# Matmul row 128 of a Fourier-MoE kernel moved to VectorE as an outer product

## The chip, the cores and the metric

The kernel runs on one core of a Trainium2 chip. The metric is the device time of one execution in microseconds. It is one program with five engines' instruction streams, ordered by semaphores that the author wrote by hand: TensorE (PE), VectorE (DVE), ScalarE (ACT), GpSimd (POOL) and SyncE (SP, which issues the DMAs).

## The reference

```
X = fft(fft(x, axis=1), axis=2).real          # x: 2 x 3008 x 256
h = X @ w_in1;  g = relu(h)**2;  y = g @ w_out1         # 256 -> 2048 -> 256
h = y @ w_in2
g = (a0 + a1*h + a2*h^2 + a3*h^3) / (1 + |b0|*|h| + |b1|*h^2 + 1e-6)
out = g @ w_out2                               # 6016 tokens
```

## The kernel before

The Fourier transform over 3008 is split into 47 and 64 points (stage 1, then `stage3` with twiddles); the transform over the 256 features is folded into `w_in1`. Tokens k and -k share their even part U and odd part V: with h1_plus = U-part and h1_minus = V-part, the two tokens' values are their sum and difference. So only 3012 columns of pairs are computed, in 12 tiles of 256 columns (`TILES`, `WIDE`; the last has 196), and each tile gives 512 tokens (the last 392).

The 128 rows of y that meet h1_plus are features 0 to 127. Feature 128 also belongs to the even part, but has no place in those 128 rows; it lies in row 0 of the odd half. Before the change it is a matmul of its own: `w_mid` and `y_mid` are 128-row tiles, zero but for three rows (weight low x y high, weight high x y high, weight high x y low). The zero rows are set by DVE (L637, L638), the three rows come by small DMAs (`load_mid`, L373, and L395), and row 0 of the odd half of `w_in1` is then zeroed by DVE (L653).

All products are done as high x high, low x high and high x low of values split in two (hi, lo), so each logical matmul is three.

The main loop has 96 steps s, 8 per tile (`UNITS`), each over two blocks of 128 of the 2048 hidden features. What the engines do in step s of the steady part, in this order:

- PE: `up1(s)` writes h1_minus (6 matmuls, L819) and h1_plus (8 matmuls, L830, two of them with w_mid) into PSUM banks 1 and 0; `down1(s-2)`; `up2(s-10)`; `down2(s-12)` (12 matmuls of 512 columns each).
- DVE: `add_and_subtract(s)` (L664, L665, reads bank 0 and the ACT copy of bank 1), `divide(s-11)` (L682, L684, L688), once in 8 steps `keep_z_lo` (L693), and `read_h2(s-10)` (L671, L672, L674).
- ACT: relu and square of unit s (L507, L509), once in 8 steps the z copy (L564), `from_h2(s-10)` (L525, L533), `keep_hi1(s)` (L516), once in 8 steps the output copy (L571), `abs_q` (L539), `keep_minus(s+1)` (L501), `seed_from_q` (L549, L552).
- POOL: `split2(s-11)` (L459, L461) and `keep_lo1(s)` (L452); before the loop it splits w_out1, w_in2 and w_out2 into hi and lo (L427, L429).
- SP: y of tiles 1 to 11 goes to DRAM in stage 3 and is read back tile by tile (L369) into one buffer, after the last `up1` of the tile before; outputs are stored.

Steps 0 to 9 lack up2 and down2 (the fill), and in them DVE also does the low part of the first g (`split1`, L703). After step 95 a tail of units without up1 is left. The last tiles of stage 3 (10 and 11) run within steps 0 and 1. `up1(m)` waits for the subtraction of m-1 (`diff_done`), `up2(m)` for `h2_read` of m-1, `add_and_subtract` for `plus_ready` and `minus_kept`.

Of the kernel before, what the change touches and what calls it, by code (L numbers as in the profile page):

```python
# [85 lines left out]
def tables():  # L86
# [43 lines left out]
def fft_moe_kernel(nc, x, w_in1, w_out1, w_in2, w_out2, coef, f47, fold, twiddle, out_t):  # L130
    y_hi_d = nc.dram_tensor("y_hi_dram", (DB, P, COLUMNS), F32, kind="Internal").ap()
    y_lo_d = nc.dram_tensor("y_lo_dram", (DB, P, COLUMNS), F32, kind="Internal").ap()

# [4 lines left out]
    with ctx:  # L138
# [42 lines left out]
        w_mid = sb("w_mid", [P, DFF], F32R)  # L181
        y_mid = sb("y_mid", [P, WIDE], F32R)
# [166 lines left out]
        def _(sp):  # L349
# [14 lines left out]
            load_w(w_out1_raw, w_out1, w_out1_loaded)  # L364

            def load_y(t):
                n = pairs(t)
                for v, s in zip(y_d, y_s):
                    sp.dma_start(s[:, :, 0:n].bitcast(F32), v[:, :, t * WIDE:t * WIDE + n]).then_inc(y_loaded, 16)  # L369

            def load_mid(t, hi, lo):
                for row, v in enumerate((hi, hi, lo)):
                    sp.dma_start(y_mid[row:row + 1, 0:pairs(t)].bitcast(F32), v).then_inc(y_mid_loaded, 16)  # L373
# [20 lines left out]
            for row, n in enumerate((1, 0, 0)):
                sp.dma_start(w_mid[row:row + 1, :].bitcast(F32), w_in1_s[n][0:1, 1, :].bitcast(F32)).then_inc(w_mid_loaded, 16)  # L395
            sp.wait_ge(y_lo_kept, 1)
            load_mid(0, *(s[0:1, 1, :].bitcast(F32) for s in y_s))
# [229 lines left out]
        def _(dve):  # L627
# [9 lines left out]
            dve.memset(w_mid[:, :].bitcast(F32), 0.0).then_inc(mid_zeroed, 1)  # L637
            dve.memset(y_mid[:, :].bitcast(F32), 0.0).then_inc(mid_zeroed, 1)  # L638
            for r in range(folds):
                sums, hi, lo = fold_views(r)  # L640
                dve.wait_ge(w_in1_hi, r + 1)
                nc.vector.tensor_tensor(lo, sums, hi.bitcast(F32), ALU.subtract).then_inc(w_in1_lo, 1)
            def keep_y_lo(t):
                hi, lo = y_tile(t)
                dve.wait_ge(y_hi_kept, t + 1)
                nc.vector.tensor_tensor(lo, uv_bank(t), hi.bitcast(F32), ALU.subtract).then_inc(y_lo_kept, 1)

            for t in range(EARLY):
# [1 line left out]
                if t == MID_AT:  # L650
                    dve.wait_ge(w_mid_loaded, 48)
                    for w in w_in1_s:
                        dve.memset(w[0:1, 1, :].bitcast(F32), 0.0).then_inc(mid_row_zeroed, 1)  # L653
# [283 lines left out]
```

## Time and profile before

| | us |
|---|---|
| median of 3 runs | 1047.09 (1045.85 to 1047.9) |
| the profiled execution | 1046.25 |
| its span, first to last instruction | 1044.5 |
| PE busy / weight loads | 1020.2 / 868.2 |
| ACT busy | 888.3 |
| DVE busy | 877.7 |
| POOL busy | 568.5 |
| mean granted TensorE clock | 0.990 |

Busy time of an engine is the union of its instructions' records. Matmuls overlap each other in the records, so how far apart two start says more than how long one is. The same holds for DVE and ACT to a smaller extent: an instruction can start a little before the record of the one ahead ends.

### The profile page before, as it was taken

How to read it: one execution, taken by the hardware profiler on the slowest of the kernel's cores; microseconds unless marked ns; L12 is line 12 of the kernel's file. 1: busy time of each engine (PE TensorE's matmuls, PEld its weight loads, DVE VectorE, ACT ScalarE, POOL GpSimd, SP SyncE). 2: the span in 40 equal slices, each digit the busy share in tenths (PEclk: the TensorE clock that was granted, in tenths of full speed). 3: DMA queues.
4: the chain of work that ended last, by engine and by line, in shares of the span. 5: the costliest groups of instructions: out<-in, count | busy, mean ns of one | idle time of the engine just before them, and what ended most of it. 6: DMA issues, size and time to landing. Idle time of an engine off the chain costs nothing.

```text
span 1044.5 us, 13875 instructions
## 1 busy us (share of the span) xinstructions
PE 1020.2 (98%) x5288; PEld 868.2 (83%) x5288; DVE 877.7 (84%) x839; ACT 888.3 (85%) x929; POOL 568.5 (54%) x303
## 2 busy tenths in 40 slices
PE   9999999999999999999999999999999999999985
PEld 8798878888888888888888888888888888888775
DVE  2455798988988988888888898898888898899997
ACT  2258888999999999999999999998998999898873
POOL 0226765565665655656556566465565565555352
PEclk9999999999999999999999999999999999999997
DMA  9765000001001001001001001001001001000000
GB/s 254 281 212 188 1 1 21 1 1 41 1 1 42 1 1 41 1 1 41 2 1 41 1 1 41 1 1 41 1 1 41 1 1 36 1 21 1 1 21 16
DMA packets 22580, 36.50 MB, mean 35 GB/s; under 512 B 1601, under 2 KB 17394, under 8 KB 21874
## 3 DMA queue, kind: packets, MB, share of 16 engines
q1 hardware_dynamic: 22514, 35.63, 10.4%
q8 instruction: 41, 0.67, 0.3%
q14 instruction: 25, 0.20, 0.1%
HBM read 23.78 MB, written 11.81 MB: 34 GB/s over the span
## 4 chain that ended last, share of the span: by engine, by line
PE 88%; DVE 6%; issue 3%; ACT 2%; DMA 0%; SPq 0%; DVEq 0%; ACTq 0%
PE ps L804 45%; PE ps L795 22%; PE ps L830 8%; PE ps L819 6%; PE ps L747 3%; PE ps L767 2%; PE ps L756 1%; DVE den_s L671 1%; DVE w_out_unsplit_lo L671 1%; DVE w_out_unsplit_lo L682 1%; DVE w_out_unsplit_lo L684 1%; DVE w_in_unsplit_hi L672 1%; ACT g_value L533 1%; PE ps L774 1%; DVE den_s L682 0%
## 5 line engine op out<-in xcount | busy, mean ns | idle before, releaser
L804 PE MATMUL ps<-g_hi,w_out_lo 128*128 128x512 f32 (+1 forms) x764 | 300.3, 393 | 15.5 <-POOL w_in_lo L461 8.8
L804 PE MATMUL ps<-g_hi,w_out_hi 128*128 128x512 f32 (+1 forms) x764 | 300.2, 393 | 0.0
L804 PE MATMUL ps<-g_lo,w_out_hi 128*128 128x512 f32 (+1 forms) x728 | 283.2, 389 | 0.0
L459 POOL CAST g_hi<-g_value 128x1024 fp32r<-128x1024 f32 x86 | 89.5, 1041 | 349.4 <-DVE g_value L688 349.4
L461 POOL TENSOR_TENSOR g_lo<-g_value,g_hi 128x1024 fp32r<-128x1024 f32 x86 | 207.6, 2414 | 6.9
L452 POOL TENSOR_TENSOR g_lo<-g_value,g_hi 128x1024 fp32r<-128x1024 f32 (+1 forms) x86 | 203.6, 2368 | 0.6 <-ACT g_hi L516 0.6
L804 PEld LDWEIGHTS ps<-g_hi,w_out_lo 128*128 128x128 f32 x764 | 145.5, 190 | 45.1 <-POOL w_in_lo L461 10.3
L804 PEld LDWEIGHTS ps<-g_hi,w_out_hi 128*128 128x128 f32 x764 | 145.1, 190 | 29.2
L671 DVE SCALAR_TENSOR_TENSOR den_s<-den_s,b_abs,ps 128x1024 f32<-128x1024 f32 x88 | 112.7, 1281 | 61.7 <-ACT g_value L533 61.5
L804 PEld LDWEIGHTS ps<-g_lo,w_out_hi 128*128 128x128 f32 x728 | 137.4, 189 | 25.5
L682 DVE SCALAR_TENSOR_TENSOR den_s<-den_s,seed_s 128x1024 f32<-128x1024 f32 x87 | 110.9, 1275 | 28.7 <-ACT seed_s L552 28.7
L539 ACT ACTIVATE den_s<-den_s 128x1024 f32<-128x1024 f32 x88 | 93.5, 1063 | 38.0 <-DVE den_s L671 38.0
L525 ACT ACTIVATE den_s<-ps,coef_s 128x1024 f32<-128x1024 f32 x88 | 98.2, 1116 | 25.9 <-PE ps L795 24.6
L795 PE MATMUL ps<-z_hi,w_in_lo 128*128 128x512 f32 x352 | 110.5, 395 | 2.9 <-DVE g_value L674 2.7
L688 DVE SCALAR_TENSOR_TENSOR g_value<-g_value,coef_s,den_s 128x1024 f32<-128x1024 f32 x86 | 110.5, 1285 | 3.0
L674 DVE SCALAR_TENSOR_TENSOR g_value<-g_value,coef_s,ps 128x1024 f32<-128x1024 f32 x86 | 110.1, 1280 | 3.0
L795 PE MATMUL ps<-z_lo,w_in_hi 128*128 128x512 f32 x352 | 109.4, 392 | 0.0
L795 PE MATMUL ps<-z_hi,w_in_hi 128*128 128x512 f32 x352 | 109.2, 392 | 0.0
L684 DVE SCALAR_TENSOR_TENSOR den_s<-den_s,seed_s 128x1024 f32<-128x1024 f32 x87 | 106.6, 1225 | 3.0
L507 ACT ACTIVATE g_value<-g_value 128x1024 f32<-128x1024 f32 (+1 forms) x96 | 100.1, 1043 | 8.2 <-DVE g_value L665 8.2
L672 DVE TENSOR_TENSOR g_value<-g_value,ps 128x1024 f32<-128x1024 f32 x86 | 104.4, 1213 | 0.0
L533 ACT ACTIVATE g_value<-ps,coef_s 128x1024 f32<-128x1024 f32 x86 | 103.3, 1201 | 0.0
(105 smaller groups left out, 1895.8 us busy)
## 6 DMA issues: line engine op xcount, KB each, us to landing
x_s<-x SPq DMA_DIRECT2D x16, 384.0 KB, 7.3
out_t<-out_s SPq DMA_DIRECT2D x11, 512.0 KB, 3.0
w_out_unsplit_lo<-w_out SPq DMA_DIRECT2D x2, 2048.0 KB, 17.7
tw_s<-twiddle SPq DMA_DIRECT2D x1, 3012.0 KB, 18.2
y_hi_dram<-y_stage_hi SPq DMA_DIRECT2D x10, 256.0 KB, 3.0
y_lo_dram<-y_stage_lo SPq DMA_DIRECT2D x10, 256.0 KB, 3.2
y_hi<-y_hi_dram SPq DMA_DIRECT2D x10, 256.0 KB, 2.8
y_lo<-y_lo_dram SPq DMA_DIRECT2D x10, 256.0 KB, 3.0
```

The source lines that it names most:

```text
L452: nc.gpsimd.tensor_tensor(g1_lo_s[:, p, :, 0:n], r_s[:, p, :, 0:n], g1_hi_s[:, m % 2, :, 0:n].bitcast(F32), ALU.subtract).then_inc(pool_lo ...
L461: nc.gpsimd.tensor_tensor(lo, g, hi.bitcast(F32), ALU.subtract).then_inc(g2_lo, 1)
L507: nc.scalar.activation(r, r, ACT.Relu).then_inc(relu_done, 1)
L533: nc.scalar.activation(num_of(m), h2_banks(m)[:, :, 0:width(m)], ACT.Identity, bias=a2, scale=a3).then_inc(cubic_done, 1)
L671: nc.vector.scalar_tensor_tensor(den, den, b_abs[:, 0:1], h2, ALU.add, ALU.mult).then_inc(q_signed, 1)
L672: nc.vector.tensor_tensor(num, num, h2, ALU.mult).then_inc(t_h_done, 1)
L674: nc.vector.scalar_tensor_tensor(num, num, a1, h2, ALU.add, ALU.mult).then_inc(h2_read, 1)
L682: nc.vector.scalar_tensor_tensor(den, den, Q_CONST, seed, ALU.add, ALU.mult).then_inc(t_done, 1)
L684: nc.vector.scalar_tensor_tensor(den, den, 2.0, seed, ALU.subtract, ALU.mult, reverse0=True).then_inc(rec_done, 1)
L688: nc.vector.scalar_tensor_tensor(num, num, a0, den, ALU.add, ALU.mult).then_inc(g2_done, 1)
L795: last = nc.tensor.matmul(h[:, i, 0:n], lhs, rhs, start=(j == 0), stop=(j == len(products) - 1))
L804: last = nc.tensor.matmul(acc[:, mb, 0:n], w[a][:, f, mb * P:(mb + 1) * P], g[c][:, i, 0:n], start=(f == 0 and j == 0), stop=(f == FB - 1 ...
```

## The change

Feature 128 leaves the matmuls. Its row of y (called u) and of w_in1 (2048 values, turned to a column of 128 per block, `w_col`) are kept in exact form; DVE writes their outer product for unit m into bank 0, and the six matmuls of h1_plus that are left add onto it (start=False).

- PE: `up1` has 6 + 6 matmuls in place of 6 + 8. Ahead of h1_minus it waits for `minus_kept` (ACT's copy), ahead of h1_plus for `outer_ready`. In stage 3, behind tile 7, one small matmul sums hi and lo of the w row into the column.
- DVE: two `tensor_scalar` of 128x256 per unit, with a per-partition scalar from `w_col`, SBUF to PSUM. They stand directly behind `add_and_subtract(s)` in steps 0 to 10, later behind `divide` and ahead of `keep_z_lo` and `read_h2`. In stage 3 a one-row copy of u per tile, ahead of the low part of y, and the copy of the column. The memsets L637, L638 and L653 go.
- POOL: two memsets of 1x2048 (the zero rows of w_in1), behind the split of w_out1 and ahead of the wait for w_in2.
- ACT: one DMA issue in stage 3.
- SP: in place of the `w_mid`/`y_mid` DMAs, two stores of the w row, one store of u per tile (1 KB), one broadcast load of u per tile to 128 partitions; y has two buffers, tile 1 is loaded at the end of stage 3 ahead of w_in2, and tile t+1 behind the last up1 of tile t-1.

```diff
+            def outer_product(m):
+                t, n = m // UNITS, pairs(m // UNITS)
+                if m % UNITS == 0:
+                    dve.wait_ge(u_loaded[t % Y_BUFS], 16 * (t // Y_BUFS + 1))
+                after(dve, diff_done, m)
+                for i in range(2):
+                    f = 2 * (m % UNITS) + i
+                    nc.vector.tensor_scalar(h1_plus(m)[:, i, :], u_s[:, t % Y_BUFS, 0:n], w_col[:, f:f + 1], None, ALU.mult
+                                            ).then_inc(outer_ready, 1)
...
                 add_and_subtract(s)
+                if before is None:
+                    outer_product(s + 1)
...
                     divide(before)
+                if before is not None and unit(s + 1) is not None:
+                    outer_product(s + 1)
                 if summed is not None and summed % UNITS == UNITS - 1:
                     keep_z_lo(summed // UNITS)
...
             def up1(m):
-                after(pe, diff_done, m)
+                after(pe, minus_kept, m)
...
-                if m % UNITS == 0:
-                    pe.wait_ge(y_mid_loaded, 48 * (t + 1))
+                pe.wait_ge(outer_ready, 2 * m + 2)
...
-                    products = [(w_in1_s[1][:, 0, f], y_s[0][:, 0, 0:n]), (w_in1_s[0][:, 0, f], y_s[1][:, 0, 0:n]),
-                                (w_mid[:, f], y_mid[:, 0:n]), (w_in1_s[0][:, 0, f], y_s[0][:, 0, 0:n])]
-                    for j, (lhs, rhs) in enumerate(products):
-                        last = nc.tensor.matmul(h1_plus(m)[:, i, :], lhs, rhs, start=(i == 0 and j == 0), stop=(j == 3),
+                    for a, c in ((1, 0), (0, 1), (0, 0)):
+                        last = nc.tensor.matmul(h1_plus(m)[:, i, :], w_in1_s[a][:, 0, f], y_s[c][:, 0, 0:n],
+                                                start=False, stop=(a, c) == (0, 0), skip_group_check=True)
...
+            pool.wait_ge(w_row_stored, 32)
+            for w in w_in1_s:
+                pool.memset(w[0:1, 1, :].bitcast(F32), 0.0).then_inc(mid_row_zeroed, 1)
...
             for t in range(1, TILES):
                 sp.wait_ge(plus_ready, t * UNITS)
-                after_stored(sp, t)
-                load_y(t)
-                load_mid(t, *(v[0:1, 1, t * WIDE:t * WIDE + pairs(t)] for v in y_d))
+                if t + 1 < TILES:
+                    load_u(t + 1)
+                    load_y(t + 1)
```

## Rows read from the trace of the kernel before

**Rows 1.** Page: engines' busy time; the chain that ended last, by engine.

```profile
PE 1020.2 (98%) x5288; PEld 868.2 (83%) x5288; DVE 877.7 (84%) x839; ACT 888.3 (85%) x929; POOL 568.5 (54%) x303
...
PE 88%; DVE 6%; issue 3%; ACT 2%; DMA 0%; SPq 0%; DVEq 0%; ACTq 0%
```

**Rows 2.** Windows: stretch, length, busy of PE, PEld, DVE, ACT, POOL; clock; DMA.

```profile
140.00:160.00 20.00, 18.09 (x80) 14.62 (x79) 17.67 (x16) 17.21 (x18) 11.70 (x7) 0.91 0.00 0
...
500.00:600.00 100.00, 99.95 (x504) 84.43 (x503) 88.90 (x83) 91.96 (x93) 57.83 (x31) 1.00 0.03 11
```

**Rows 3.** PE by form, then timeline (start, duration) of two successive steps.

```profile
L830 PE MATMUL ps<-y_mid,w_mid 128*128 128x256 f32 x176 | 49.1, 279 | 0.0
...
609.92 0.28 PE L830 MATMUL ps<-y_mid,w_mid 128*128 128x256 f32 x1
610.04 0.28 PE L830 MATMUL ps<-y_hi,w_in_hi 128*128 128x256 f32 x1
...
619.85 0.28 PE L830 MATMUL ps<-y_mid,w_mid 128*128 128x256 f32 x1
```

**Rows 4.** DVE timeline, steady steps, one with z; idle before in brackets.

```profile
499.08 1.28 DVE L671 SCALAR_TENSOR_TENSOR den_s<-den_s,b_abs,ps 128x1024 f32<-128x1024 f32 x1 [0.92 <-ACT g_value L533]
...
504.28 1.23 DVE L682 SCALAR_TENSOR_TENSOR den_s<-den_s,seed_s 128x1024 f32<-128x1024 f32 x1 [0.26 <-ACT seed_s L552]
...
506.80 1.28 DVE L688 SCALAR_TENSOR_TENSOR g_value<-g_value,coef_s,den_s 128x1024 f32<-128x1024 f32 x1
508.00 1.22 DVE L693 TENSOR_TENSOR z_lo<-ps,z_hi 128x1024 fp32r<-128x1024 f32 x1
509.98 1.28 DVE L671 SCALAR_TENSOR_TENSOR den_s<-den_s,b_abs,ps 128x1024 f32<-128x1024 f32 x1 [0.76 <-ACT g_value L533]
...
519.37 1.28 DVE L671 SCALAR_TENSOR_TENSOR den_s<-den_s,b_abs,ps 128x1024 f32<-128x1024 f32 x1 [0.40 <-ACT g_value L533]
```

**Rows 5.** DVE timeline in the tail: a short instruction with per-partition scalar.

```profile
1033.76 0.63 DVE L688 SCALAR_TENSOR_TENSOR w_in_unsplit_hi<-w_in_unsplit_hi,coef_s,w_out_unsplit_lo 128x392 f32<-128x392 f32 x1
1034.30 0.97 DVE L698 TENSOR_TENSOR w_in_hi<-w_in_unsplit_hi,g_hi 128x784 fp32r<-128x784 f32 x1
```

**Rows 6.** DVE timeline: a 256-wide memset; two 512-wide instructions without such a scalar.

```profile
38.06 0.27 DVE L638 MEMSET y_mid<- 128x256 f32 x1
...
502.73 0.68 DVE L664 TENSOR_TENSOR g_value<-ps,minus_s 128x512 f32<-128x512 f32 x1
503.33 0.68 DVE L665 TENSOR_TENSOR g_value<-ps,minus_s 128x512 f32<-128x512 f32 x1
```

**Rows 7.** DVE timeline: an L682 while GpSimd still works.

```profile
464.60 1.27 DVE L682 SCALAR_TENSOR_TENSOR den_s<-den_s,seed_s 128x1024 f32<-128x1024 f32 x1 [0.26 <-ACT seed_s L552]
465.91 1.23 DVE L684 SCALAR_TENSOR_TENSOR den_s<-den_s,seed_s 128x1024 f32<-128x1024 f32 x1
```

**Rows 8.** DVE timeline, steps of the narrow last tile.

```profile
944.76 1.28 DVE L671 SCALAR_TENSOR_TENSOR den_s<-den_s,b_abs,ps 128x1024 f32<-128x1024 f32 x1 [0.17 <-ACT g_value L533]
...
949.86 1.25 DVE L682 SCALAR_TENSOR_TENSOR den_s<-den_s,seed_s 128x1024 f32<-128x1024 f32 x1 [0.42 <-ACT seed_s L552]
...
952.40 1.28 DVE L688 SCALAR_TENSOR_TENSOR g_value<-g_value,coef_s,den_s 128x1024 f32<-128x1024 f32 x1
953.93 1.28 DVE L671 SCALAR_TENSOR_TENSOR den_s<-den_s,b_abs,ps 128x1024 f32<-128x1024 f32 x1 [0.24 <-ACT g_value L533]
```

**Rows 9.** Timelines of the fill: ACT's copy in two steps; PE's wait for tile 1.

```profile
85.77 0.58 ACT L501 ACTIVATE minus_s<-ps 128x512 f32<-128x512 f32 x1
...
89.88 0.58 ACT L501 ACTIVATE minus_s<-ps 128x512 f32<-128x512 f32 x1
...
102.50 0.39 PE L819 MATMUL ps<-y_hi,w_in_lo 128*128 128x256 f32 x1 [0.69 <-DMA y_lo<-y_lo_dram]
```

**Rows 10.** GpSimd timeline: end of the w_out1 split, start and end of the later splits.

```profile
57.77 2.35 POOL L429 TENSOR_TENSOR w_out_lo<-w_out_unsplit_lo,w_out_hi 128x1024 fp32r<-128x1024 f32 x1
87.27 1.04 POOL L427 CAST w_in_hi<-w_in_unsplit_lo 128x1024 fp32r<-128x1024 f32 x1 [27.15 <-DMA w_in_unsplit_lo<-w_in]
...
119.12 2.40 POOL L429 TENSOR_TENSOR w_out_lo<-w_out_unsplit_lo,w_out_hi 128x1024 fp32r<-128x1024 f32 x1
```

More of the change, by code:

```diff
@@ L48 @@
 MID_AT = 3
+Y_BUFS = 2
 WIDE = 2 * BATCH * N2
@@ L127, in column_of_token, with fft_moe_kernel @@
     return column
-def fft_moe_kernel(nc, x, w_in1, w_out1, w_in2, w_out2, coef, f47, fold, twiddle, out_t):
+def fft_moe_kernel(nc, x, w_in1, w_out1, w_in2, w_out2, coef, f47, fold, twiddle, pair, out_t):
     y_hi_d = nc.dram_tensor("y_hi_dram", (DB, P, COLUMNS), F32, kind="Internal").ap()
     y_lo_d = nc.dram_tensor("y_lo_dram", (DB, P, COLUMNS), F32, kind="Internal").ap()
+    u_d = nc.dram_tensor("u_dram", (1, COLUMNS), F32, kind="Internal").ap()
+    w_row_d = nc.dram_tensor("w_row_dram", (2, DFF), F32, kind="Internal").ap()
     out_v = out_t.rearrange("(k p) n -> p k n", p=P)
@@ L179, in kept_and_rest @@
             return value, sb(f"{name}_lo", [P, bufs, 2, TN], F32R)
-        w_mid = sb("w_mid", [P, DFF], F32R)
-        y_mid = sb("y_mid", [P, WIDE], F32R)
+        u_s = sb("u_s", [P, Y_BUFS, WIDE])
+        w_rows = sb("w_rows", [2 * FB, P])
+        pair_s = sb("pair_s", [2 * FB, FB])
+        w_col = sb("w_col", [P, FB])
+        with ExitStack() as transform:
+            u_stage = sb("u_stage", [1, STAGE_BUFS + 1, WIDE], stack=transform)
+        y_odd = [sb(f"y_odd_{n}", [P, DB, WIDE], F32R) for n in ("hi", "lo")]
+        sb("to_w_in2", [P, DFF + WIDE - Y_BUFS * WIDE - 2 * DB * WIDE - P - 2 * FB])
         w_in2_s, (_, w_in2_raw) = weights("w_in2", [P, DB, DFF])
@@ L364, in _, with store_u, load_u @@
             load_w(w_out1_raw, w_out1, w_out1_loaded)
+            after(sp, s1_ready, S1_GROUPS)
+            sp.dma_start(pair_s[:, :], pair).then_inc(pair_loaded, 16)
             def load_y(t):
                 n = pairs(t)
[L368 to L373, printed above, removed]
+                for v, s in zip(y_d, y_of(t)):
+                    sp.dma_start(s[:, :, 0:n].bitcast(F32), v[:, :, t * WIDE:t * WIDE + n]
+                                 ).then_inc(y_loaded[t % Y_BUFS], 16)
+            def store_u(t):
+                n = t % (STAGE_BUFS + 1)
+                sp.wait_ge(u_kept, t + 1)
+                sp.dma_start(u_d[:, t * WIDE:t * WIDE + pairs(t)], u_stage[:, n, 0:pairs(t)]).then_inc(u_stored[n], 16)
+            def load_u(t):
+                n = pairs(t)
+                after_u_stored(sp, t)
+                sp.dma_start(u_s[:, t % Y_BUFS, 0:n], u_d[:, t * WIDE:t * WIDE + n].to_broadcast([P, n])
+                             ).then_inc(u_loaded[t % Y_BUFS], 16)
             def store_out(t):
@@ L390, in store_y @@
                                  ).then_inc(y_stored[(t - 1) % STAGE_BUFS], 16)
-            sp.wait_ge(mid_zeroed, 2)
             sp.wait_ge(w_in1_lo, folds)
[L394 to L397, printed above, removed]
+            for n in range(2):
+                sp.dma_start(w_row_d[n:n + 1, :], w_in1_s[n][0:1, 1, :].bitcast(F32)).then_inc(w_row_stored, 16)
+            store_u(0)
             for t in range(1, TILES):
+                store_u(t)
                 store_y(t)
+                if t <= Y_BUFS:
+                    load_u(t - 1)
             for t in range(TILES - STAGE_BUFS, TILES):
                 after_stored(sp, t)
+            for t in range(TILES - STAGE_BUFS - 1, TILES):
+                after_u_stored(sp, t)
+            load_y(1)
             load_w(w_in2_raw, w_in2, w_in2_loaded)
@@ L649, in _ @@
                 keep_y_lo(t)
[L650 to L653, printed above, removed]
+                if t == COLUMN_AT + 1:
+                    dve.wait_ge(w_col_summed, 1)
+                    nc.vector.tensor_copy(w_col[:, :], ps[:, FOLD_BANKS[2], 0:FB]).then_inc(w_col_ready, 1)
+                    dve.wait_ge(w_col_ready, 1)
+                    outer_product(0)
             dve.wait_ge(coef_loaded, 16)
@@ L786, in _ @@
                 stage3(t)
+                if t == COLUMN_AT:
+                    pe.wait_ge(w_in1_lo, folds)
+                    pe.wait_ge(pair_loaded, 16)
+                    pe.wait_ge(w_rows_loaded, 16)
+                    nc.tensor.matmul(ps[:, FOLD_BANKS[2], 0:FB], w_rows[:, :], pair_s[:, :], start=True, stop=True
+                                     ).then_inc(w_col_summed, 1)
             def up(h, w, src, m, n, ready):
```

33 lines of the change are left out of this document (23 added, 10 removed).

## Prediction

> **What bounds the kernel now.** I read the page first: PE is busy in 98% of the span and makes up 88% of the chain that ended last, against 84% and 85% for DVE and ACT [rows 1]. Then the windows: from about 160 to 900 us PE is busy all the time (99.95 of 100 us at clock 1.00), DVE 88.9, ACT 92.0 [rows 2]. Then the timelines, for the spacing. The same matmul of two successive steps starts 9.93 us apart (9.92 over many steps), and two neighbours of 256 columns 0.12 us apart [rows 3]. DVE shows how near the next limit is. From L671 to L682 it takes 5.20 us (through ACT's abs, copy, ln and exp), from L682 to L688 2.52, and behind L688 the next instruction starts 1.20 later if nothing holds it: 8.92 us. Then it waits for ACT before L671, 0.92 us in the usual step [rows 4]. ACT's own loop, where it is not held by PE, brings L671 every 9.39 us (509.98 to 519.37) [rows 4]. So there are three rings side by side: PE 9.92, ACT 9.39, and DVE with ACT's seed in it 8.92. The tail behind step 95 is DVE's, back to back, and the change adds nothing there.
>
> **What goes on PE.** Two of 14 short matmuls per unit, 192 in all (176 of them 256 wide) [rows 3]. 2 x 0.12 = 0.24 us per step: PE's ring becomes 9.68. The wait that moved from the subtraction to ACT's copy comes earlier than the old one, so it costs nothing.
>
> **What comes on DVE, and where.** Two `tensor_scalar` of 256 columns with a per-partition scalar stand between L688 and L671, so they lie in the 8.92 ring, not beside it. The 0.92 us of waiting before L671 covers them only until the ring is longer than PE's. No row shows such an instruction, nor any DVE write to PSUM. What one takes of DVE's time is the distance to the next start. For instructions with such a scalar it is 1.20 us at 1024 columns [rows 4] and 0.54 at 392 [rows 5], so 1.044 ns per column, and 0.54 - 136 x 0.001044 = 0.40 us at 256. Without the scalar 512 columns take 0.60 [rows 6]; by the same slope 256 take 0.33. The low end is the memset of 256 columns, which reads nothing: 0.27 [rows 6]. The high end is a PSUM write that takes away the overlap with the next instruction: the 0.63 record at 392 [rows 5] less 0.14 gives 0.49. So the pair costs 0.54 to 0.98, and I take 0.80, from the nearest rows in kind (same scalar operand, same engine).
>
> One rule of the Trainium skill bears on it. Its page "Vector Engine (DVE) Microarchitecture Reference", section "Measured stream behaviour on trn2", gives 1.0417 ns per column and about 75 ns per instruction, whatever the op; that is an estimate of 0.34 each, 0.68 the pair. The slope agrees with this trace, but the rows with a per-partition scalar show some 0.06 us more.
>
> **Steady steps.** DVE's ring is 8.92 + 0.80 = 9.72, against PE's 9.68: DVE takes over as the bound. Once in 8 steps z_lo stands in the same ring; its record is 1.22 [rows 4], its slot 0.08 less, 1.14. The mean is 9.72 + 1.14/8 = 9.86, against 9.92: 0.06 us gained per step. The z copy of ACT (about 0.9) and its output copy (0.3 late at L539 now) run beside the longer DVE part and cost nothing more. PE's phase changes too: up2 of the next unit waits for L674, which ends 3.73 after L671, and the way from there round PE is 9.68, so it is no ring of its own. Another edge is GpSimd: where L682 comes early behind the L688 before, it overlaps the last GpSimd subtraction and takes 1.27, and L684 starts 1.31 later in place of 1.26 [rows 7]. That was 7.08 us behind L688; with 0.80 it is 1.20 + 0.80 + 5.20 = 7.20, so about nothing; with 0.67 it is 7.07 and costs 0.05 per step. 96 steps less 14 of fill and 8 narrow ones are 74: -4.4 us.
>
> **Narrow tile.** Steps now take 9.17 (944.76 to 953.93). DVE's ring: 5.10 + 2.54 [rows 8] + 1.20, and two instructions of 196 columns, 0.34 each: 9.52. Six steps lose 0.34, 2.0 us; the first and the one with z_lo gain about 0.3 together. +1.7 us.
>
> **Fill.** Steps 1 to 10 are PE's: ten times 0.24 gained, if ACT's loop lets it. That brings the minus copy every 4.11 us [rows 9], against PE's 4.46 now and 4.22 after, so it just does. DVE has over a microsecond idle per step there; the pair hides. The second y buffer takes away PE's wait of 0.69 us for tile 1 [rows 9]; later tiles' loads were hidden anyway. -3.1 us. Then two steps (10 to 12) are already ruled by the ACT ring of 9.39 and will be by DVE's 9.72: +0.7. The w column's small matmul stands on PE in stage 3, about 0.3 (one matmul behind a wait took 0.39 [rows 9]). Hidden: the DVE memsets that go (PE had other work), the row copies of u (DVE idles 1.1 us per tile in stage 3), and SP's extra issues, some 1.7 us per tile of stage 3 against 1.79 that PE gives it. GpSimd ends the w_out1 split at 60.1 us [rows 10]; two memsets of 2048 columns, 1.8 each on DVE, end near 64, ahead of the first up1 at 66.7. The w_in2 load is issued some 1 us later and shares the DMA engines with tile 1, so the split that starts at 87.3 and ends at 121.5 [rows 10] ends 2 to 3 us later; PE needs it at 123 to 125 and has waits for `h2_read` behind it that take up what is left. Sum of the start: -2.1 us.
>
> The clock was granted at 0.91 over 140 to 160 us [rows 2], about 2 us lost in a stretch at the lower level behind a wait of PE; I leave it as it is, within 2 us either way.
>
> **Sum.** -4.4 + 1.7 - 2.1 = -4.8 us. Against the profiled execution's 1046.25 that is 1041.5; the median of the runs is 0.84 above it, so 1042.3. I say 1042. Each 0.01 us on the pair moves it by 0.8 us; from 0.86 on nothing is gained.
>
> **Rivals.**
> - The pair costs as instructions without a scalar, 0.67. Ring 9.59 and 0.05 for GpSimd, with z_lo 9.78: -0.14 x 74 = -10.4; narrow +1.3, start -2.3: 1035.7. For it: the same slope, and one tensor input less. Against: all three kinds of rows with a scalar are dearer.
> - PE stays the bound: the pair is 0.62 or less ((9.68 - 1.14/8) - 8.92), as it would be if one instruction did two columns per cycle (0.40 less 0.13 is 0.27 each, 0.53). -0.24 x 74, narrow -1.8, start -2.8: 1024.7. For it: the memset's 0.27. Against: no row of DVE is faster than one column per cycle but by a few per cent. The skill's page "VectorE: DVE Perf Modes", section "The perf-mode tier table", gives fp32 `tensor_scalar` twice the rate in SBUF, and not with an operand in PSUM; where that cap did not hold for the destination, this would be the result.
> - Slower: a write to PSUM does not overlap the next instruction. The pair is 0.98, the ring 9.90, with z_lo 10.04: +0.12 x 74 = +8.9; narrow 9.68 a step, +2.8; start -1.7: 1057. It decides from 0.88 per pair. For it: nothing in the trace shows a PSUM write by DVE. Against: reading PSUM or SBUF makes no difference to the distance (L671 and L688 both 1.20).
> - The zero rows on GpSimd are late, or the split of w_in2 is: if a memset of one row took four times DVE's 1.8 us, up1(0) would start at 74 and not at 66.7. With the rest as forecast: 1049.
>
> **How the numbers follow.** What a measurement of this kernel can tell from no change is about 0.2%, 2.1 us. Forecast 0.44, pair as without scalar 0.24, PE-bound 0.07, slower by the PSUM write 0.15, late start 0.03; the rest, 0.07, is a pair between 0.83 and 0.88. Faster: 0.24 + 0.07 + 0.39 = 0.70; same 0.12 (that rest and the upper edge of the forecast); slower 0.18. The range goes from 1030 to 1053: it holds the forecast, the cheaper pair, and the near half of the slower case, and leaves out PE-bound and the dearest pairs. The likeliest case's own range is 1039 to 1045.
>
> **What would show it.** In the steady steps: L671 without idle time ahead of it (0.92 to about 0), 9.7 us between two of them and 10.86 across a z_lo; the two new instructions at 0.40 us distance; PE idle 0.05 to 0.2 us per step, released by DVE's outer product or by L674, and busy no longer 99.9%. Up1 with 12 matmuls in 1.43 us. In the fill no wait for y_lo at tile 1, and first up2 done some 3 us sooner. In the narrow tile 9.5 us per step. A pair at 0.34 us distance or less, or PE without idle time, would show the forecast wrong on the fast side; more than 0.43, on the slow side.

## The result, and the profile after

| | before | after |
|---|---|---|
| median, us | 1046.7 (1045.42 to 1047.9, 8 runs) | 1043.12 (1040.07 to 1044.19, 8 runs) |
| ratio | | 0.9961 [0.9947, 0.9975] |
| the profiled execution / its span | 1046.25 / 1044.5 | 1043.1 / 1041.3 |

The forecast was 1042. The time fits, but partly by luck: two of its terms are wrong by 6.1 and 4.7 us, with opposite signs. Most of what follows is about them.

In the kernel after, L671, L672, L674 are L725, L726, L728; L664 and L665 are L718 and L719; L682, L684, L688 are L736, L738, L742; `keep_z_lo` is L747 and the outer product L690. PE's up1 is L884 and L892, up2 L859, down L868. GpSimd's split of g is L498, L500, L491, its split of the weights L463, L465; ACT's L533 is L575.

The page (busy time by engine, then the chain by engine) answers to [rows 1]: PE 17 us less, DVE 64 more, and the chain is no longer PE's.

```profile
PE 1003.2 (96%) x5098; PEld 848.1 (81%) x5098; DVE 941.8 (90%) x1040; ACT 882.0 (85%) x929; POOL 572.1 (55%) x305
...
DVE 45%; ACT 28%; issue 15%; PE 9%; POOL 2%; DMA 1%; DVEq 0%; ACTq 0%; SPq 0%
```

Windows (columns as in [rows 2]). The first is a stretch in which PE now stands still; the others answer to [rows 2].

```profile
120.00:140.00 20.00, 12.98 (x52) 10.41 (x51) 18.11 (x16) 15.84 (x18) 16.19 (x9) 0.74 0.00 0
140.00:160.00 20.00, 20.00 (x101) 16.91 (x100) 17.60 (x21) 16.81 (x18) 11.58 (x6) 1.00 0.00 1
500.00:600.00 100.00, 98.66 (x486) 82.58 (x485) 96.23 (x103) 91.82 (x95) 59.04 (x31) 1.00 0.05 13
```

DVE's timeline in two steady steps, the second with a z_lo; it answers to [rows 4]. The two halves of the outer product are one row (x2).

```profile
486.75 1.28 DVE L742 SCALAR_TENSOR_TENSOR g_value<-g_value,coef_s,den_s 128x1024 f32<-128x1024 f32 x1
487.95 0.87 DVE L690 TENSOR_SCALAR ps<-u_s,w_col 128x256 f32<-128x256 f32 x2
488.73 1.27 DVE L725 SCALAR_TENSOR_TENSOR den_s<-den_s,b_abs,ps 128x1024 f32<-128x1024 f32 x1
...
493.91 1.23 DVE L736 SCALAR_TENSOR_TENSOR den_s<-den_s,seed_s 128x1024 f32<-128x1024 f32 x1 [0.27 <-ACT seed_s L594]
...
498.41 1.27 DVE L725 SCALAR_TENSOR_TENSOR den_s<-den_s,b_abs,ps 128x1024 f32<-128x1024 f32 x1
...
508.10 1.21 DVE L747 TENSOR_TENSOR z_lo<-ps,z_hi 128x1024 fp32r<-128x1024 f32 x1
509.23 1.27 DVE L725 SCALAR_TENSOR_TENSOR den_s<-den_s,b_abs,ps 128x1024 f32<-128x1024 f32 x1
```

From L690 to L725 it is 0.78 us: the pair's price. L725 has no idle time ahead of it (0.92 before), and steps are 9.68 to 9.70 apart, 10.82 across the z_lo. A tile of eight steps takes 78.7 us, where it took 79.6.

PE's own spacing must be read beside this. In the usual step the first matmul of up1 starts 9.70 us after that of the step before (mean of these steps, 170 to 885 us), so PE and DVE are equally long. Once per tile PE plainly waits for DVE: the z_lo makes L728 late, and up2 of the next tile waits for it. In most tiles this step is 10.74 on PE, and the two starts at the wait are 1.07 apart in place of 0.23 (PE's timeline of the kernel after):

```profile
590.75 0.40 PE L868 MATMUL ps<-g_hi,w_out_hi 128*128 128x512 f32 x1
591.82 0.47 PE L859 MATMUL ps<-z_hi,w_in_lo 128*128 128x512 f32 x1 [0.67 <-DVE g_value L728]
```

The whole difference can be laid out on one instruction. In the two traces the first instruction of `read_h2` of steps 13, 87 and 94 and of the last unit starts at (before: L671, after: L725):

```profile
150.75 1.28 DVE L671 SCALAR_TENSOR_TENSOR den_s<-den_s,b_abs,ps 128x1024 f32<-128x1024 f32 x1 [1.33 <-ACT g_value L533]
887.36 1.28 DVE L671 SCALAR_TENSOR_TENSOR den_s<-den_s,b_abs,ps 128x1024 f32<-128x1024 f32 x1 [0.92 <-ACT g_value L533]
...
1026.71 1.02 DVE L671 SCALAR_TENSOR_TENSOR w_out_unsplit_lo<-w_out_unsplit_lo,b_abs,ps 128x784 f32<-128x784 f32 x1
```

```profile
154.79 1.28 DVE L725 SCALAR_TENSOR_TENSOR den_s<-den_s,b_abs,ps 128x1024 f32<-128x1024 f32 x1
882.34 1.27 DVE L725 SCALAR_TENSOR_TENSOR den_s<-den_s,b_abs,ps 128x1024 f32<-128x1024 f32 x1
949.87 1.27 DVE L725 SCALAR_TENSOR_TENSOR den_s<-den_s,b_abs,ps 128x1024 f32<-128x1024 f32 x1
1022.62 1.03 DVE L725 SCALAR_TENSOR_TENSOR w_out_unsplit_lo<-w_out_unsplit_lo,b_abs,ps 128x784 f32<-128x784 f32 x1
```

(Step 94 before: 953.93, in [rows 8].)

| stretch | before | after | difference | forecast |
|---|---|---|---|---|
| start, to step 13 | 150.75 | 154.79 | +4.0 | -2.1 |
| 74 steady steps | 736.61 | 727.55 | -9.1 | -4.4 |
| narrow steps, 87 to 94 | 66.57 | 67.53 | +1.0 | +1.7 |
| behind that, to the end of the span | 90.6 | 91.4 | +0.9 | 0 |
| span | 1044.5 | 1041.3 | -3.2 | -4.8 |

**The start, up to step 10.** The first `read_h2` (step 10) starts at 121.21 before and at 121.22 after, where the forecast had it 2.8 us earlier (3.1 for the fill less 0.3 for the column's matmul). The first up1 starts 1.19 later: stage 3 began 0.67 later (49.59 in place of 48.92; in the other versions, whose code is the same up to there, it begins at 49.19 to 50.18), and the column's matmul takes about 0.4 of PE. The next three steps, with the last two tiles of stage 3 in them, take 13.66 in place of 12.58. DVE works from 74.4 to 82.6 us without a gap, with the pair and the copies of u added, and PE waits for it twice:

```profile
76.62 0.39 PE L892 MATMUL ps<-y_hi,w_in_lo 128*128 128x256 f32 x1 [0.64 <-DVE ps L690]
78.66 0.50 PE L868 MATMUL ps<-g_hi,w_out_lo 128*128 128x512 f32 x1 [1.06 <-DVE g_lo L757]
```

From there to up1 of step 10 the forecast holds: 30.07 in place of 32.22.

**The start, from step 10 on.** DVE, GpSimd and PE between 124 and 135 us of the kernel after (start, duration; idle before in brackets):

```profile
126.41 1.97 DVE L736 SCALAR_TENSOR_TENSOR den_s<-den_s,seed_s 128x1024 f32<-128x1024 f32 x1 [0.27 <-ACT seed_s L594]
128.41 3.25 DVE L738 SCALAR_TENSOR_TENSOR den_s<-den_s,seed_s 128x1024 f32<-128x1024 f32 x1
131.69 1.28 DVE L742 SCALAR_TENSOR_TENSOR g_value<-g_value,coef_s,den_s 128x1024 f32<-128x1024 f32 x1
132.90 0.87 DVE L690 TENSOR_SCALAR ps<-u_s,w_col 128x256 f32<-128x256 f32 x2
```

```profile
124.91 2.38 POOL L465 TENSOR_TENSOR w_out_lo<-w_out_unsplit_lo,w_out_hi 128x1024 fp32r<-128x1024 f32 x1
127.25 3.32 POOL L491 TENSOR_TENSOR g_lo<-g_value,g_hi 128x1024 fp32r<-128x1024 f32 x1
```

```profile
133.82 0.58 PE L892 MATMUL ps<-y_odd_hi,w_in_lo 128*128 128x256 f32 x1 [5.50 <-DVE ps L690]
```

Two things meet here. GpSimd's weight split, which ended at 121.5 before [rows 10], now ends at 127.3, in the middle of the first `divide`. L736 and L738 both read two tensors in SBUF, as do L465 and L491, and none of the two on DVE gets done while one of the two on GpSimd is at work: L736 lasts 0.74 us longer than its usual 1.23 and ends 1.1 behind L465, L491 lasts 3.32 in place of 2.4, and L738 3.25, ending 1.1 behind L491. And the outer product of unit 12 is the first that stands behind a `divide` in place of directly behind the subtraction, so PE, which needs it for up1 in step 12, stands still for 5.5 us with the down products queued behind (just ahead of this it had already waited 1.52 us for L465); the granted clock is 0.74 in that window, and behind the wait the matmuls of 256 columns start 0.21 apart in place of 0.12: the lower of the two levels, 1.2 GHz.

The Trainium skill, page "SBUF — State Buffer", section "Who interferes with whom", has this as a rule: a VectorE instruction with two SBUF inputs and a GpSimd instruction that reads SBUF exclude each other for the whole of an instruction, and whoever is issued first goes on. The four rows agree with it.

### The profile page after: what moved, and what is told of

It reads as the page before. It is cut to its first block, busy times and chain, and to the rows that moved or that the text cites. A ratio compares the mean times of both kernels' runs of the same rounds, so it can differ in the third digit from the quotient of the medians.

```text
span 1041.3 us, 13708 instructions
## 1 busy us (share of the span) xinstructions
PE 1003.2 (96%) x5098; PEld 848.1 (81%) x5098; DVE 941.8 (90%) x1040; ACT 882.0 (85%) x929; POOL 572.1 (55%) x305
## 4 chain that ended last, share of the span: by engine, by line
DVE 45%; ACT 28%; issue 15%; PE 9%; POOL 2%; DMA 1%; DVEq 0%; ACTq 0%; SPq 0%
DVE den_s L725 9%; DVE den_s L738 9%; DVE den_s L736 9%; ACT seed_s L594 9%; ACT seed_s L591 8%; DVE g_value L742 8%; ACT minus_s L543 5%; DVE ps L690 4%; PE ps L805 3%; PE ps L825 2%; PE ps L814 1%; ACT g_value L575 1%; PE ps L868 1%; ACT g_value L549 1%; POOL w_in_lo L465 1%
## 5 line engine op out<-in xcount | busy, mean ns | idle before, releaser
L868 PE MATMUL ps<-g_hi,w_out_lo 128*128 128x512 f32 (+1 forms) x764 | 301.6, 395 | 17.3 <-POOL w_in_lo L500 8.0
L868 PE MATMUL ps<-g_hi,w_out_hi 128*128 128x512 f32 (+1 forms) x764 | 300.3, 393 | 0.0
L868 PE MATMUL ps<-g_lo,w_out_hi 128*128 128x512 f32 (+1 forms) x728 | 283.9, 390 | 0.0
L498 POOL CAST g_hi<-g_value 128x1024 fp32r<-128x1024 f32 x86 | 89.6, 1042 | 339.5 <-DVE g_value L742 339.5
L500 POOL TENSOR_TENSOR g_lo<-g_value,g_hi 128x1024 fp32r<-128x1024 f32 x86 | 207.3, 2411 | 6.9
L491 POOL TENSOR_TENSOR g_lo<-g_value,g_hi 128x1024 fp32r<-128x1024 f32 (+1 forms) x86 | 204.6, 2380 | 0.0
L868 PEld LDWEIGHTS ps<-g_hi,w_out_lo 128*128 128x128 f32 x764 | 145.9, 191 | 47.3 <-POOL w_in_lo L500 9.3
L868 PEld LDWEIGHTS ps<-g_hi,w_out_hi 128*128 128x128 f32 x764 | 145.2, 190 | 29.2
L868 PEld LDWEIGHTS ps<-g_lo,w_out_hi 128*128 128x128 f32 x728 | 137.9, 189 | 25.6
L736 DVE SCALAR_TENSOR_TENSOR den_s<-den_s,seed_s 128x1024 f32<-128x1024 f32 x87 | 107.7, 1238 | 25.3 <-ACT seed_s L594 25.3
L859 PE MATMUL ps<-z_hi,w_in_lo 128*128 128x512 f32 x352 | 110.7, 395 | 8.4 <-DVE g_value L728 8.4
L725 DVE SCALAR_TENSOR_TENSOR den_s<-den_s,b_abs,ps 128x1024 f32<-128x1024 f32 x88 | 112.1, 1273 | 5.3 <-ACT g_value L575 5.0
L742 DVE SCALAR_TENSOR_TENSOR g_value<-g_value,coef_s,den_s 128x1024 f32<-128x1024 f32 x86 | 110.5, 1285 | 3.0
L728 DVE SCALAR_TENSOR_TENSOR g_value<-g_value,coef_s,ps 128x1024 f32<-128x1024 f32 x86 | 110.2, 1281 | 3.0
L738 DVE SCALAR_TENSOR_TENSOR den_s<-den_s,seed_s 128x1024 f32<-128x1024 f32 x87 | 108.6, 1249 | 3.0
L859 PE MATMUL ps<-z_lo,w_in_hi 128*128 128x512 f32 x352 | 109.0, 391 | 0.0
L859 PE MATMUL ps<-z_hi,w_in_hi 128*128 128x512 f32 x352 | 108.6, 390 | 0.0
L726 DVE TENSOR_TENSOR g_value<-g_value,ps 128x1024 f32<-128x1024 f32 x86 | 104.5, 1215 | 0.0
L575 ACT ACTIVATE g_value<-ps,coef_s 128x1024 f32<-128x1024 f32 x86 | 103.1, 1199 | 0.0
## 6 DMA issues: line engine op xcount, KB each, us to landing
w_in_raw<-w_in SPq DMA_DIRECT2D x1, 2048.0 KB, 10.5
```

The source lines that it names most:

```text
L491: nc.gpsimd.tensor_tensor(g1_lo_s[:, p, :, 0:n], r_s[:, p, :, 0:n], g1_hi_s[:, m % 2, :, 0:n].bitcast(F32), ALU.subtract).then_inc(pool_lo ...
L500: nc.gpsimd.tensor_tensor(lo, g, hi.bitcast(F32), ALU.subtract).then_inc(g2_lo, 1)
L575: nc.scalar.activation(num_of(m), h2_banks(m)[:, :, 0:width(m)], ACT.Identity, bias=a2, scale=a3).then_inc(cubic_done, 1)
L725: nc.vector.scalar_tensor_tensor(den, den, b_abs[:, 0:1], h2, ALU.add, ALU.mult).then_inc(q_signed, 1)
L726: nc.vector.tensor_tensor(num, num, h2, ALU.mult).then_inc(t_h_done, 1)
L728: nc.vector.scalar_tensor_tensor(num, num, a1, h2, ALU.add, ALU.mult).then_inc(h2_read, 1)
```

## Experiments

All changes are against the kernel after. Each ratio is against a before measured in the same series: 1047.31 for the load moved, the pair moved in every step, 14 matmuls and the pair twice; 1046.51 for the others. Where a time is set against the kernel after (1043.12), the two come from different series, whose befores lie within 0.8 us.

### The load of w_in2 ahead of tile 1

```diff
@@ SP, end of stage 3
+            load_w(w_in2_raw, w_in2, w_in2_loaded)
+            load_w(w_out2_raw, w_out2, w_out2_loaded)
             load_y(1)
-            load_w(w_in2_raw, w_in2, w_in2_loaded)
-            load_w(w_out2_raw, w_out2, w_out2_loaded)
```

> SP issues the loads of w_in2 and w_out2 ahead of the load of y tile 1; all else as changed. Theory A (the start is lost by the late split of w_in2 and w_out2 on GpSimd, which ends at 127.3 us where it ended at 121.5 before, holds DVE in the first divide for 2.8 us and then PE for 5.5): the w_in2 load is issued 1 us earlier and doesn't share its time with y; it landed 6.3 us later than before, of which 2.9 come from the last store of y and remain. The split ends at about 124.5; the first L742 comes about 2 us earlier; 1040 to 1042, 1 to 3 us faster than the changed kernel. Rival B (the load's lateness comes from stage 3 ending late alone): no difference. Rival C: y of tile 1 now comes late and PE waits for it: it is needed at 102 us and would land at about 98, so no.

Measured 1038.08 (1037.21 to 1039.16), ratio 0.9914 [0.99, 0.9927]: more than theory A's 1040 to 1042. The load of w_in2 is issued only 0.3 us earlier (83.33), but the split starts at 90.77 in place of 93.60 and ends at 125.3; step 13's L725 comes at 152.94, 1.85 earlier than in the kernel after. DVE's timeline: L736 still meets the end of L491 (at 127.67), L738 is free.

```profile
127.26 1.49 DVE L736 SCALAR_TENSOR_TENSOR den_s<-den_s,seed_s 128x1024 f32<-128x1024 f32 x1 [0.27 <-ACT seed_s L594]
128.78 1.23 DVE L738 SCALAR_TENSOR_TENSOR den_s<-den_s,seed_s 128x1024 f32<-128x1024 f32 x1
```

PE still waits, 4.78 us, for the outer product:

```profile
132.16 0.58 PE L892 MATMUL ps<-y_odd_hi,w_in_lo 128*128 128x256 f32 x1 [4.78 <-DVE ps L690]
```

So the late split is one part of the start's loss: PE's 1.52 us for L465 is gone and the wait of 5.50 is 0.72 shorter, but most of that wait stays. The span is 3.9 us shorter, and 1.9 of that is this. The other 2.0 lies behind the last L725, where nothing was changed and the clock was higher (0.86 from 1020 to 1040 us, 0.66 after the change). Whether that is chance stays open: all four runs here show a mean clock of 0.992 or 0.993, and only two of the eight of the kernel after show 0.992, at 1040.1 and 1040.3 us. So the 5.0 us between the medians is explained for 1.9.

### The outer product directly behind the subtraction in every step

```diff
                 add_and_subtract(s)
-                if before is None:
+                if unit(s + 1) is not None:
                     outer_product(s + 1)
...
-                if before is not None and unit(s + 1) is not None:
-                    outer_product(s + 1)
```

> The outer product stands directly behind add_and_subtract in every step, not behind divide. Theory A (the steady step is DVE's ring L725 to L725, 8.91 + 0.78 = 9.69): DVE waits there 0.27 us for ACT's seed, and behind the difference the pair begins 0.1 later because it waits for its end; the way from L725 to L736 becomes 4.23 + 0.72 + 0.78 = 5.73 in place of 5.19 and the pair is gone from the rest, 9.45 in all, with z_lo 9.59: less than PE's 9.68. PE is the bound, -0.16 us x 74 steps and some in the narrow tile: 1030 +- 3. Rival (PE is the bound already, and its 9.68 is met by the 9.69): no change, 1043. Rival (the position matters since PE gets its outer product too late): the same gain, but then PE's idle time before up1 in the changed kernel would be seen behind the outer product, and the trace shows it behind L728.

Measured 1033.57 (1033.07 to 1034.18), ratio 0.987 [0.9857, 0.9884], just above the range of 1030 +- 3. PE's long wait is gone, and DVE's usual steady steps are 9.64 apart: the pair now runs while ACT makes the seed for L736, where DVE had waited 0.27. DVE's timeline of a steady step, and GpSimd's of the same:

```profile
566.18 0.68 DVE L719 TENSOR_TENSOR g_value<-ps,minus_s 128x512 f32<-128x512 f32 x1
566.90 0.88 DVE L690 TENSOR_SCALAR ps<-u_s,w_col 128x256 f32<-128x256 f32 x2
567.68 1.40 DVE L736 SCALAR_TENSOR_TENSOR den_s<-den_s,seed_s 128x1024 f32<-128x1024 f32 x1
569.12 1.23 DVE L738 SCALAR_TENSOR_TENSOR den_s<-den_s,seed_s 128x1024 f32<-128x1024 f32 x1
```

```profile
565.58 2.43 POOL L491 TENSOR_TENSOR g_lo<-g_value,g_hi 128x1024 fp32r<-128x1024 f32 x1
```

The expected ring of 9.45 isn't reached: L736 would come before L491 ends at 568.0, and lasts 1.40 until 1.1 behind that. L742 releases GpSimd's split of g, and the split's last part holds L736: with DVE it forms a ring of its own, of 9.64. That is less than PE's spacing, 9.69 in seven of eight steps, so PE is the bound in those, as theory A had it. The 4.9 us that 74 steady steps gain (722.7 in place of 727.6) come for the most part from the step with the z_lo: on PE it takes 10.2 to 10.5 now, where it took 10.74 in most tiles.

### Both

The two edits together.

> Loads of w_in2 and w_out2 ahead of y tile 1, and the outer product directly behind the difference in every step. If the two gains are of different places (start, steady steps) they add: 1043 - 5 - 9.5 = 1028.5. If both mend the same loss at the start (DVE's first divide held by GpSimd's late split, and PE waiting for the outer product behind it), part is counted twice: 1031 to 1033. Steady steps as in the run with the product behind the difference, 9.64 with L736 at 1.40 us.

Measured 1031.23 (1030.91 to 1031.95), ratio 0.9854 [0.984, 0.9867]: the fastest complete version, and faster than before and after. The first `divide` is no longer held, and the window in which PE stood still reads:

```profile
120.00:140.00 20.00, 18.52 (x94) 15.29 (x93) 18.28 (x20) 18.85 (x20) 12.78 (x7) 1.00 0.00 1
```

From the first L725 to that of step 13 the traces show 29.5 us before, 33.6 after, 30.9 with the load moved, 30.9 with the pair moved, 28.7 with both. So each edit takes away 2.7 and both together 4.9: nearly additive in this stretch, and the two causes account for all of the 4.0 that it had lost. They do nothing for the 2.8 that failed to be gained ahead of it (first L725 at 121.43). Steady steps are as with the pair moved alone (722.7 us for 74). The time as a whole is not additive (1028.5 was expected for that). In the traces most of what is missing lies behind step 94, where the load moved is 2.0 shorter than the kernel after, the pair moved 0.5, and both 1.0.

### Only unit 12's outer product moved

```diff
-                if before is None:
+                if before is None or before == 0:
                     outer_product(s + 1)
...
-                if before is not None and unit(s + 1) is not None:
+                if before is not None and before > 0 and unit(s + 1) is not None:
```

> Only the outer product of unit 12 (step 11) goes directly behind the difference instead of behind the first divide; all else as changed. Theory (PE waits 5.5 us there since this product stands behind the first divide, which waits for the first seed and for GpSimd; the clock then falls): PE's wait goes, the clock stays at 1.00 in 120 to 140 us, 2 to 4 us gained, 1039 to 1041; the steady steps unchanged at 9.69. Rival (the start is bound by GpSimd's late split in any case): PE waits for GpSimd instead, under 1 us gained.

Measured 1040.78 (1039.81 to 1041.63), ratio 0.9945 [0.9933, 0.9957]. PE's 5.5 us wait splits into smaller ones (1.8 for the weight split, 1.3 for L491, 1.4 for the outer product of unit 13, which still stands behind its `divide`), the clock in 120 to 140 us is still 0.83, and the stretch from the first L725 to step 13 is 32.0 in place of 33.6. The rest of the wait had only been covered by it: L738 is held for 3.27 here too. Moving one instance takes 1.6 us; moving those behind it too takes 2.7 with the split just as late (the run with every pair moved). The time is the one expected, but the theory's own signs, no wait of PE and a clock of 1.00, are not there: the rival is right that PE then waits for GpSimd, though it had the gain at under 1 us.

### Two of the removed matmuls back on PE

```diff
-                    for a, c in ((1, 0), (0, 1), (0, 0)):
+                    for a, c in ((1, 0), (1, 0), (0, 1), (0, 0)):
```

One product per block is added twice, so h1_plus is wrong by that product; PE has 14 short matmuls per unit as before.

> As changed, but one of the six h1_plus products per block is issued twice, so PE has 14 short matmuls per unit again (the low-by-high product is added twice). Theory A: PE's ring is 9.92 again against DVE's 9.69 (9.83 with z_lo): PE the bound, 0.09 us x 74 = +6.5 us against the changed kernel, 1049 to 1051. Then the kernel's gain in the steady part needs both sides, and DVE takes the pair in for nothing. Rival (DVE's pair is the cost of the step and PE's work is beside it): no difference, 1043.

Measured 1052.93 (1052.65 to 1053.25), ratio 1.0055 [1.0041, 1.0069], 9.8 us above the kernel after and above the 1049 to 1051 of theory A. Windows and DVE's timeline:

```profile
500.00:600.00 100.00, 99.98 (x502) 84.44 (x501) 95.55 (x103) 91.39 (x94) 58.36 (x30) 1.00 0.04 13
```

```profile
503.02 0.87 DVE L690 TENSOR_SCALAR ps<-u_s,w_col 128x256 f32<-128x256 f32 x2
504.03 1.28 DVE L725 SCALAR_TENSOR_TENSOR den_s<-den_s,b_abs,ps 128x1024 f32<-128x1024 f32 x1
```

PE is the bound again: steps of 9.93, a tile of 79.7 (79.6 before), and 0.23 us of slack between the pair and L725. So the pair is nearly hidden in the steady part as long as PE has 14 matmuls (737.8 us for 74 steps, 736.6 before), and the 9 us that the steady part gained come from the two matmuls. It cost more than the 6 to 8 expected for the same reason that the forecast's steady term was too small (below).

### The pair twice

Each `tensor_scalar` is issued a second time with the same operands, behind a wait for its first issue; only the second signals PE.

> As changed, but each of the two tensor_scalar is issued twice (same result). Theory A: ring 9.69 + 0.78 + a little for the wait = 10.5 to 10.55; +0.8 x 82 steps: +66 us, 1106 to 1112. Rival (PE is still the bound, DVE has slack of some tenths): +0.78 less the slack; with 0.1 of slack +58 us or less.

Measured 1108.09 in one run. L690 and the repeated L695 start at 507.05 and 507.83, the next L730 (this kernel's `read_h2`) at 508.60; steps are 10.46 apart, 9.69 plus 0.77. What is added on DVE in this place adds the same to the step, with nothing to hide it. Together with the 14 matmuls this says that neither engine has slack in the kernel after: more work on either makes the step longer.

### No pair

```diff
-                for i in range(2):
+                for i in range(0):
...
-                pe.wait_ge(outer_ready, 2 * m + 2)
+                after(pe, diff_done, m)
...
-                                                start=False, stop=(a, c) == (0, 0), skip_group_check=True)
+                                                start=(i == 0 and (a, c) == (1, 0)), stop=(a, c) == (0, 0), skip_group_check=True)
```

Feature 128's product is left out altogether, and PE's first product starts the sum.

> As changed without the two tensor_scalar (feature 128's product is left out of the result); PE waits for the subtraction ahead of h1_plus instead. Theory A: DVE's ring is 8.91, PE the bound at 9.68 with no idle time: 0.16 us x 74 below the changed kernel, narrow tile 0.3 x 6 too, and PE has no wait of 5.5 us in step 12: 1043 - 12 - 2 - 3 = 1026. It is the floor for any place of the pair. Rival (something else holds the steady step at 9.69): 1040.

Measured 1031.78 (1031.48 to 1031.9), ratio 0.9858 [0.9844, 0.9871]. The floor of 1026 is not there. From the first L725 to step 13 it takes 32.3 us, 2.7 more than before: without any pair, the late split still holds L738 for 3.27, and PE waits 1.67 and 1.61 for GpSimd. The steady part gains 5.7 where 12 was expected, because PE's step with the z_lo stays at 10.2 (9.69 in the others). DVE's timeline has slack again, and two steps are still 9.70 apart:

```profile
483.92 1.28 DVE L725 SCALAR_TENSOR_TENSOR den_s<-den_s,b_abs,ps 128x1024 f32<-128x1024 f32 x1 [0.52 <-ACT g_value L575]
...
493.62 1.28 DVE L725 SCALAR_TENSOR_TENSOR den_s<-den_s,b_abs,ps 128x1024 f32<-128x1024 f32 x1 [0.57 <-ACT g_value L575]
```

That is PE's ring with 12 short matmuls, forecast at 9.68. The 74 steady steps take 721.9 us, against 722.7 with the pair directly behind the subtraction: there the pair is all but free, and moving it gets back 4.9 of the 5.7 us that the pair costs the steady part in its place behind the `divide`. This run also shows what the pair costs in the fill: up1 of step 3 starts 12.56 us behind the first one, and 13.66 in the kernel after.

### The pair as one instruction

```diff
-                for i in range(2):
-                    f = 2 * (m % UNITS) + i
-                    nc.vector.tensor_scalar(h1_plus(m)[:, i, :], u_s[:, t % Y_BUFS, 0:n], w_col[:, f:f + 1], None, ALU.mult
-                                            ).then_inc(outer_ready, 1)
+                f = 2 * (m % UNITS)
+                nc.vector.tensor_tensor(h1_plus(m), u_s[:, t % Y_BUFS, 0:n].unsqueeze(1).to_broadcast([P, 2, n]),
+                                        w_col[:, f:f + 2].unsqueeze(2).to_broadcast([P, 2, n]), ALU.mult
+                                        ).then_inc(outer_ready, 2)
```

> The two tensor_scalar become one tensor_tensor of 2x256 (u repeated over the blocks, the column value repeated along the row), at the same place behind divide. Theory A1 (only the sum on DVE counts): 0.60 us as other 512-wide rows in place of 0.78, ring 9.51, 1.5 us per tile: -14, PE-bound at about 1031. Theory A2 (an instruction with two SBUF inputs shuts GpSimd's reads out and is shut out by them, as L736 was at 1.40 us in the run with the product behind the difference): GpSimd's cast starts 1.35 behind L742 and now waits for the tensor_tensor until 1.80, its chain of 5.85 us ends at 7.65 and not at 7.20, and L736, ready at 6.99, lasts 1.8 us: ring 9.65 to 9.7, no gain. A broadcast operand that is read slower would show as a record above 0.68.

Measured 1062.02 (1061.28 to 1064.41), ratio 1.0145 [1.0129, 1.016]: slower than either theory. The instruction itself is the cheaper one. DVE's and GpSimd's timelines:

```profile
489.07 0.69 DVE L689 TENSOR_TENSOR ps<-u_s,w_col 128x512 f32<-128x512 f32 x1
489.68 1.27 DVE L725 SCALAR_TENSOR_TENSOR den_s<-den_s,b_abs,ps 128x1024 f32<-128x1024 f32 x1
...
494.87 1.73 DVE L736 SCALAR_TENSOR_TENSOR den_s<-den_s,seed_s 128x1024 f32<-128x1024 f32 x1 [0.27 <-ACT seed_s L594]
```

```profile
489.22 1.44 POOL L498 CAST g_hi<-g_value 128x1024 fp32r<-128x1024 f32 x1 [3.73 <-DVE g_value L742]
490.74 2.41 POOL L500 TENSOR_TENSOR g_lo<-g_value,g_hi 128x1024 fp32r<-128x1024 f32 x1
493.12 2.40 POOL L491 TENSOR_TENSOR g_lo<-g_value,g_hi 128x1024 fp32r<-128x1024 f32 x1
```

It takes 0.61 us in place of 0.78. But it has two inputs in SBUF and starts 0.15 us ahead of GpSimd's cast, which waits it out (1.44 in place of 1.04); L491 ends at 495.5 and not at 494.0 as in the kernel after (0.9 of the 1.5 because the whole step lies that much later), and L736, which needs two SBUF inputs too, lasts 1.73 until 1.1 behind it. The step is 10.03: 0.17 saved, 0.51 lost. Theory A2 named this mechanism and nearly the record (1.8), but its terms don't add up to its sum: 6.99 until L736 is ready, 1.8 for it and 1.26 for L738 make 10.05, and not 9.65 to 9.7.

## Why the prediction came out, point by point

- **The pair, 0.80.** Right: 0.78, 0.39 each. The rival without scalar cost (0.67) and the one with no overlap after a PSUM write (0.98) are both refuted; a 256-column `tensor_scalar` to PSUM overlaps the next instruction as others do.
- **DVE takes over, ring 9.72.** Right for DVE's ring: 9.69, with L725 following L690 at once, and 10.82 across z_lo (forecast 10.86). But PE's, forecast at 9.68, is 9.69 too. In the usual step neither bounds alone: the pair twice adds 0.77, and two more matmuls on PE add 0.24. What DVE costs beyond PE comes once per tile, at the z_lo, so spreading z_lo as 1.14/8 over all steps gave about the right mean in the wrong place.
- **Steady gain, -4.4.** Mis-sized: -9.1. The step after was forecast at 9.86 and is 9.83, which is 2 us of it. The rest is the baseline. I took 9.92 for before, but 736.61 us for 74 steps are 9.954. Once per tile PE lost about 0.27 us, where z_lo made L674 late for up2. PE's waits between 170 and 900 us list none of it, since the record ahead covers it; only the starts show it, 0.42 apart where they are 0.23 elsewhere, and the step across them on PE, 10.2 in place of 9.92 (PE's timeline of the kernel before, L804's last matmul and the L795 behind it):

```profile
513.20 0.40 PE L804 MATMUL ps<-g_lo,w_out_hi 128*128 128x512 f32 x1
513.43 0.40 PE L804 MATMUL ps<-g_hi,w_out_hi 128*128 128x512 f32 x1
513.85 0.70 PE L795 MATMUL ps<-z_hi,w_in_lo 128*128 128x512 f32 x2
```

- **GpSimd's edge, about nothing.** Right for this order: L736 lasts 1.23. With GpSimd 0.4 us later behind L742 (1.73) the edge is what bounds; with the pair ahead of L736 (1.40) it holds DVE, but PE's 9.69 is the longer.
- **Narrow steps.** 9.46 where 9.52 was forecast; +1.0 in all against +1.7.
- **The start, -2.1.** Wrong: +4.0, a term off by 6.1 us, 2.8 of them ahead of step 10 and 3.3 behind. Some parts were right: no wait for `y_lo` at tile 1, the 0.24 per step from step 3 on, and the two memsets on GpSimd, which took 1.80 and 1.79 and stayed hidden. Ahead of step 10 the sentence "DVE has over a microsecond idle per step there; the pair hides" failed: in steps 2 and 3 DVE has no idle time, and the pair costs 1.1 us up to there. The first up1 came at 67.89 and not at 66.70; the w column's small matmul is about 0.4 of that (forecast 0.3), and stage 3 began 0.67 later, the cause of which is open. Behind step 10 two more steps failed. "Ends 2 to 3 us later" for the split: it ended 5.8 later, since the load was issued 3.9 later, behind tile 1's, and landed 6.3 later. And "PE needs it at 123 to 125 and has waits for `h2_read` behind it that take up what is left" looked at PE alone; the split holds DVE's two-input instructions as well, which was in [rows 7] and in the edge named for the steady part, but not applied here. Further, I let the outer product join the steady ring from step 10 on and didn't ask who waits for the very first one behind a `divide`: PE, with the down products queued behind its wait.
- **The clock, left as it was.** The stretch at the lower level moved and grew: 120 to 140 us went from 1.00 to 0.74, and 140 to 160 us from 0.91 to 1.00. This is part of the start's loss, as it follows PE's long wait.
- **Behind the narrow steps, 0.** +0.9 in the one profile of each. From the last `read_h2` to the end of the span it takes 17.8 us before and 18.7 after, and 16.7 to 18.9 in the other versions, with PE at times on the lower clock; not settled.

The sum was within 2 us by luck, because +6.1 and -4.7 met. The late-start rival, given 0.03, was in effect the case that happened, in another form and next to a larger gain.

## What to carry to other kernels

Work put on an engine that is about to become the bound belongs where that engine waits for another (here between the subtraction and the seed), not at the end of its chain; the same two instructions cost 5.7 us or 0.8 over 74 steps. Two inputs in SBUF on VectorE are a resource shared with GpSimd: an instruction that is shorter but has two can cost more than it saves by pushing GpSimd into the next one (here 0.17 saved and 0.51 lost per step). A baseline per step is to be taken over whole periods (here 74 steps or a tile), because the chosen "usual" step leaves out what happens once per period.

## What the hardware showed that was not expected

- The exclusion between a VectorE instruction with two SBUF inputs and GpSimd is not a slowdown in proportion: the one waits to the end of the other, and ended 1.1 us behind it whatever the wait was (1.40, 1.73, 1.97 and 3.25 us records of instructions that take 1.23). Both engines pay it: 1.44 for a cast of 1.04, and 3.32 for a subtraction of 2.4.
- After PE's wait of 5.5 us the matmuls of 256 columns started 0.21 us apart, and the stretch had a granted clock of 0.74; with waits of at most 2.3 us in 100 to 160 us (pair and load moved) it stayed at 1.00. The longest wait alone doesn't tell, though: in the kernel before, where none there was above 1.9 us, it was 0.91 from 140 to 160 us [rows 2].
- A `tensor_tensor` of 512 columns with both inputs repeated by the access pattern, one of them an innermost scalar, takes 0.61 us, no more than a plain one [rows 6].
- GpSimd's memset of one row of 2048 takes 1.80 us, about the value that the forecast had taken over from DVE.
